# Attention and two feed-forward layers on one core: planes of probabilities in three buffers, casts and value products a step later

## What is computed

```python
scores = q @ k.T / sqrt(D) + bias(pos)     # per head
attn = exp(scores - max); attn = attn / (sum(attn) + 1e-9)
x = attn @ v                               # heads side by side: 2304 x 512
h = x @ w_in;  x = (s * relu(h)**2 + b) @ w_out
h = x @ w2_in; out = (h - tanh(h)) @ w2_out
```

## Time and profile before

| | us |
|---|---|
| median of 3 runs | 1117.99 |
| profiled execution | 1118.78 |
| its span | 1117.0 |
| TensorE matmul busy | 1055.4 (94%) |
| ScalarE busy | 728.8 (65%) |
| GpSimd (POOL) busy | 681.0 (61%) |
| VectorE busy | 622.2 (56%) |

### The profile page before, as it was taken

How to read it: one execution, slowest core, us unless ns; L and a number is a source line. 1 busy time by engine, 2 the same in 40 slices (tenths; PEclk the granted TensorE clock), 3 DMA queues, 4 the chain that set the end, 5 groups by cost and what they waited for, 6 DMA issues and landing times.

```text
span 1117.0 us, 16823 instructions
## 1 busy us (share of the span) xinstructions
PE 1055.4 (94%) x5668; PEld 912.4 (82%) x5668; DVE 622.2 (56%) x1120; ACT 728.8 (65%) x1477; POOL 681.0 (61%) x656
## 2 busy tenths in 40 slices
PE   4669999899999999999999999999999999999998
PEld 1158887778888888888888878888888888999998
DVE  6868876655775376458765754672361361450540
ACT  8968886666777587668776876784463463563552
POOL 1045674478678667767776778666455455555453
PEclk9989999999999999999999999999999999999999
DMA  4778875599779787988897899765333234333332
GB/s 164 248 237 254 282 212 143 146 223 252 207 189 263 220 202 198 260 201 208 225 247 187 208 229 236 209 159 142 115 97 114 94 114 131 112 113 113 95 122 81
DMA packets 185481, 202.49 MB, mean 181 GB/s; under 512 B 125954, under 2 KB 128692, under 8 KB 185396
## 3 DMA queue, kind: packets, MB, share of 16 engines
q1 hardware_dynamic: 185108, 201.35, 65.4%
q10 hardware_dynamic: 288, 0.07, 0.0%
HBM read 156.55 MB, written 15.64 MB: 154 GB/s over the span
## 4 chain that ended last, share of the span: by engine, by line
PE 58%; ACT 15%; issue 8%; DMA 8%; DVE 7%; SPq 2%; POOL 1%; ACTq 0%; DVEq 0%; POOLq 0%
PE ps_f L888 16%; PE ps_f L890 16%; PE ps_f L889 16%; DMA p_t<-planes 6%; ACT planes L608 3%; ACT x_raw L331 2%; DVE g_buf L948 2%; DVE g_buf L951 2%; ACT gh L901 1%; ACT ps_s L620 1%; PE ps_s L561 1%; ACT stage L348 1%; PE ps_o L520 1%; PE ps_o L535 1%; DVE planes L727 1%
## 5 line engine op out<-in xcount | busy, mean ns | idle before, releaser
L845 POOL TENSOR_TENSOR wl<-w_raw,wh 128x512 fp32r<-128x512 f32 x318 | 417.0, 1316 | 289.1 <-ACT wh L838 288.4
L888 PE MATMUL ps_f<-gh,wh 128*128 128x464 f32 (+1 forms) x640 | 243.1, 380 | 1.9 <-DVE g_buf L948 1.4
L888 PE MATMUL ps_f<-xh,wh 128*128 128x464 f32 (+1 forms) x640 | 241.0, 377 | 3.7 <-DVE g_buf L948 1.9
L890 PE MATMUL ps_f<-xh,wl 128*128 128x464 f32 (+1 forms) x640 | 237.7, 371 | 0.0
L889 PE MATMUL ps_f<-xl,wh 128*128 128x464 f32 (+1 forms) x640 | 237.5, 371 | 0.0
L889 PE MATMUL ps_f<-gl,wh 128*128 128x464 f32 (+1 forms) x640 | 237.3, 371 | 0.0
L890 PE MATMUL ps_f<-gh,wl 128*128 128x464 f32 (+1 forms) x640 | 237.1, 370 | 0.0
L838 ACT ACTIVATE wh<-w_raw 128x512 fp32r<-128x512 f32 x318 | 196.4, 623 | 45.7 <-PE ps_f L890 41.5
L888 PEld LDWEIGHTS ps_f<-xh,wh 128*128 128x128 f32 x640 | 120.7, 189 | 17.9 <-DVE g_buf L948 2.9
L888 PEld LDWEIGHTS ps_f<-gh,wh 128*128 128x128 f32 x640 | 120.9, 189 | 15.6 <-DVE g_buf L948 2.6
L890 PEld LDWEIGHTS ps_f<-xh,wl 128*128 128x128 f32 x640 | 120.4, 188 | 13.5
(11 more groups left out here) (107 smaller groups left out, 1695.5 us busy)
## 6 DMA issues: line engine op xcount, KB each, us to landing
w_raw<-in_w_out SPq DMA_DIRECT2D x80, 512.0 KB, 3.5
w_raw<-in_w_in SPq DMA_DIRECT2D x79, 512.0 KB, 3.5
bias_t<-bias_flat SPq DMA_DIRECT2D x128, 288.0 KB, 4.0
bias_flat<-stage SPq DMA_DIRECT2D x36, 295.5 KB, 2.2
k_raw<-in_kt SPq DMA_DIRECT2D x32, 288.0 KB, 3.9
q_raw<-in_qt SPq DMA_DIRECT2D x32, 288.0 KB, 3.5
v_raw<-in_vt SPq DMA_DIRECT2D x32, 288.0 KB, 3.3
bias_t<-bias_flat SPq DMA_DIRECT2D x32, 144.0 KB, 3.6
```

Source lines behind the costliest of these rows:

```text
L845: pool.tensor_tensor(wl[:, b % RING, :, :], raw_block(b), wh[:, b % RING, :, :].bitcast(F32), ALU.subtract).then_inc(w_lo_done, 1)
L888: pe.matmul(acc, hi, rhs_h[:, k0 + kk, 0:T], start=(first and kk == 0), stop=False)
L890: mm = pe.matmul(acc, lo, rhs_h[:, k0 + kk, 0:T], start=False, stop=(last and kk == 3))
```

## The change

- The scores of head 10 get SBUF homes, `p_even` and `p_odd`, in the space that the last rows of `gh` and `gl` take up later. Their planes are made in the step after, as for the other heads, and their scores wait for the row minimum alone.
- There are three plane buffers for the later heads: `planes` (two, over the dead `ptl`) and `plane_c` (over the dead `inv_b`). The low parts that head 9's tiles still need go to `ptl_late`, over `y`.
- `cast` and `valued` come a step later for tiles from 50 on, so there is one step more in all.
- SP sends the first plane of a head after all value products of head h - 2 but the last, and after the last cast of that head.
- RAW is 3: a third weight buffer. SP's loads run one pair further ahead, and a third pair is loaded at step (7, 2) of the part that runs alone.

```diff
RING = 4
-RAW = 2
+RAW = 3
 AHEAD = 3
...
     TILES = BH * NT
-    STEPS_AT = list(range(TILES + NT + 2))
+    STEPS_AT = list(range(TILES + NT + 3))
     FIRST = (H + 1) * NT + 1 + EXTRA
...
         p_lo_done = sem("p_lo_done")
-        plane_turned = [sem(f"plane_turned{i}") for i in range(2)]
+        plane_turned = [sem(f"plane_turned{i}") for i in range(3)]
         block_cast = sem("block_cast")
...
         pth = tile("pth", [P, 2, S], F32R)
-        ptl = tile("ptl", [P, 2, S], F32R)
+        with nc.sbuf_tensor("ptl", [P, 2, S], F32R) as ptl:
+            pass
+        planes = tile("planes", [P, 2, 2 * S], F16)
         o_tmp = tile("o_tmp", [D, 2, HALF])
...
         inv_row = tile("inv_row", [NT, P])
-        inv_b = tile("inv_b", [P, S])
+        with nc.sbuf_tensor("inv_b", [P, S], F32) as inv_b:
+            pass
+        plane_c = tile("plane_c", [P, 2 * S], F16)
         x_raw = tile("x_raw", [P, KD, RINGX])
...
             pass
+        with nc.sbuf_tensor("gh_head", [P, KF - 2, TMAX], F32), nc.sbuf_tensor("p_even", [P, S], F32) as p_even:
+            pass
         gh = tile("gh", [P, KF, TMAX], F32R)
+        with nc.sbuf_tensor("gl_head", [P, KF - 2, TMAX], F32), nc.sbuf_tensor("p_odd", [P, S], F32) as p_odd:
+            pass
         gl = tile("gl", [P, KF, TMAX], F32R)
+        with nc.sbuf_tensor("ptl_late", [P, 2, S], F32R) as ptl_late:
+            pass
         y = tile("y", [P, KD, TMAX])
...
-        planes = tile("planes", [P, 2, 2 * S], F16)
         def carve(home, parts):
...
-            if FIRST_PLANE <= g < FIRST_PLANE + NT:
-                return g
-            return g - 1 if FIRST_PLANE + NT < g <= TILES else None
+            return g - 1 if FIRST_PLANE < g <= TILES else None
+        def plane_home(f):
+            first = f - FIRST_PLANE
+            return first % 2 if first < 2 * NT else (first + 1) % 3
+        def plane_uses(home, f):
+            return len([e for e in range(FIRST_PLANE, f) if plane_home(e) == home])
...
-            return planes[:, f % 2, :]
+            home = plane_home(f)
+            return planes[:, home, :] if home < 2 else plane_c[:]
...
-            for par in range(2):
-                count = len([f for f in range(FIRST_PLANE, (n + 1) * NT) if f % 2 == par])
-                eng.wait_ge(plane_turned[par], count * DMA)
+            for home in range(3):
+                need(eng, plane_turned[home], plane_uses(home, (n + 1) * NT) * DMA)
...
             R = ROWS[i % NT]
-            return pth[P - R:P, slot(i), :] if R < P else ptl[:, slot(i), :]
+            return pth[P - R:P, slot(i), :] if R < P else low_parts(i)
+        def low_parts(i):
+            return (ptl if i < FIRST_PLANE - NT else ptl_late)[:, slot(i), :]
...
-            return g - NT - 1 if FIRST_PLANE <= g - NT - 1 < TILES else None
+            return g - NT - 2 if FIRST_PLANE <= g - NT - 2 < TILES else None
...
-            return g - NT - 2 if 0 <= g - NT - 2 < TILES else None
+            if g - NT - 2 < FIRST_PLANE:
+                return g - NT - 2 if g >= NT + 2 else None
+            return g - NT - 3 if FIRST_PLANE <= g - NT - 3 < TILES else None
...
                 if u < NT - 1:
-                    mm = pe.matmul(ps_o[:, half, 0:HALF], vhl[:, n % 2, u, :], ptl[:, slot(i), cols],
+                    mm = pe.matmul(ps_o[:, half, 0:HALF], vhl[:, n % 2, u, :], low_parts(i)[:, cols],
                                    start=False, stop=False)
...
                 pe.wait_ge(back_done, PACKS - 2 if t == 0 else PACKS)
-            elif n < TURNED or n == TURNED and t == 0:
+            elif n <= TURNED:
                 pe.wait_ge(min_done, n * NT + t)
-            elif n == TURNED:
-                pe.wait_ge(p_lo_done, t)
             else:
...
             need(pe, inv_row_done, v)
-            if v + 1 < TURNED:
-                pe.wait_ge(min_done, (v + 1) * NT + 3)
-            else:
-                pe.wait_ge(p_lo_done, 3)
+            pe.wait_ge(min_done, (v + 1) * NT + 3)
             pe.transpose(ps_s[0:NT, 0, HALF:HALF + P], inv[:], ident[:]).then_inc(inv_turned, 1)
...
-            return halves(p_t[:, n % 2, t, :]) if n < TURNED else score_bank(n, t)[:, :, 0:HALF]
+            if n < TURNED:
+                return halves(p_t[:, n % 2, t, :])
+            if n == TURNED:
+                return halves((p_odd if t % 2 else p_even)[:])
+            return score_bank(n, t)[:, :, 0:HALF]
...
             act.wait_ge(scale_done, f - FIRST_PLANE + 1)
-            need(act, plane_turned[f % 2], (f - FIRST_PLANE) // 2 * DMA)
+            need(act, plane_turned[plane_home(f)], plane_uses(plane_home(f), f) * DMA)
             act.activation(halves(plane(f)[:, 0:S]), score_home(n, t), ACT.Copy, scale=inv_n[:, t:t + 1])\
...
             f = planes_of(g)
-            if f is not None and f < g:
+            if f is not None:
                 act_plane(act, f)
...
                     .then_inc(sum_done, 1)
-                if f == g:
-                    act_plane(act, f)
             if t == 0 and turning(n):
...
             n, t = divmod(f, NT)
-            if f < FIRST_PLANE + 2:
-                dve.wait_ge(pv_done, FIRST_PLANE - NT - 1)
             dve.wait_ge(p_hi_done, f - FIRST_PLANE + 1)
...
             i, j, f = turned(g - alone), valued(g), planes_of(g)
-            if f is not None and f < g:
+            if f is not None:
                 dve_scale(dve, f)
...
                     .then_inc(min_done, 1)
-            if f == g:
-                dve_scale(dve, f)
             if f is not None:
...
                     else:
-                        sp.wait_ge(pv_done, (h - 1) * NT)
+                        sp.wait_ge(pv_done, (h - 1) * NT - 1)
+                        sp.wait_ge(block_cast, (h - 1) * NT - FIRST_PLANE)
                 R = ROWS[at]
                 sp.dma_start_transpose(turned_planes(h)[:, :, P * at:P * at + R], plane(f)[0:R, :])\
-                    .then_inc(plane_turned[f % 2], DMA)
+                    .then_inc(plane_turned[plane_home(f)], DMA)
             if t == 0 and turning(n - 1):
...
                 n, t = divmod(g, NT)
-                if t == 2 and n in (3, 5):
+                if t == 2 and n in (3, 5, 7):
                     sp_weights(sp, (n - 1) // 2)
```

## The result

The changed kernel takes 1100.09 us (median of 4 runs, 1098.85 to 1102.39), where the kernel before took 1117.94 beside it: a ratio of 0.9844, interval 0.9823 to 0.9865. That is 17.9 us less; 24 were forecast. The profiled execution took 1100.6 us, its span 1098.8.

A forecast was written before the change was run, and what follows sets the result against it. TensorE was taken to lose 34 us, in head 10's serial chain and in dense stretches waiting for landings and casts. Gains 9 + 16 less 0.5 (port) and 0.5 (SP) made 24: 1094 us, own range 1090 to 1099, wide range 1088 to 1107.

The forecast's parts named there:

- Head 10: Five row-minimum intervals of VectorE take 44.23 us where 33.4 would do; 9 of the 10.9 us gained, ends 6 and 10.9.
- The collision on VectorE: Head 10's second planes read two SBUF tiles, sharing ports with GpSimd: at most 3.9 us on VectorE, 0.5 charged.
- The dense stretches: Five stretches with attention steps between weight blocks: 16 of 20 us gained, bounds 6 and 20, limited by the DMA.
- The chain from ScalarE's wait at 338.06 to TensorE's at 346.04: ScalarE's 1.88 us landing wait makes wh, wl and POOL's cast late, so TensorE's value product waits 1.56 us.
- Three plane buffers: ScalarE overwrites a buffer after three steps, not two; its 35.3 us of landing waits, costing TensorE through others, should go.
- Casts a step later: First cast two steps after a head's last plane; POOL's 8.9 us of landing waits and TensorE's behind it go, cost nothing.
- The third weight buffer: Weight loads get two blocks (5 to 7 us) more slack; attention-only phase cost 0, bounds -0.5 to +2 us.
- SP's wait for the cast: SP's first plane of a head delayed 0.8 us per head; 0.5 us charged in all, bound 16 us.
- rival A: The DMA queue is the bound and buffers only move the wait; landings lengthen to 8 or 9 us: 1103, chance 0.15.

The follow-up runs named there:

- a1_head10: Changed kernel with everything but head 10's part taken back (two plane and two weight buffers, old cast and value steps, SP's old wait): 1109.8 us, ratio 0.9915.
- c1_before_light: Kernel before the change, loading only a quarter of each bias row from head 11 on (result not the reference's, for time alone): 1113.5 us, ratio 0.996.
- a4_cast_early: Changed kernel with casts and value products back in their old steps, three plane and three weight buffers kept: 1108.5 us, ratio 0.9911.
- b1_cast_first: Changed kernel with POOL's cast ahead of its split of k in the first step of a head: 1097.5 us, ratio 0.981.
- a2_two_planes: Changed kernel with two plane buffers in place of three: 1103.9 us, ratio 0.9866.
- b2_scale_late: Changed kernel with POOL's last scaling of two heads a step later, behind the first cast of head 10: 1099.2 us, ratio 0.9826.
- a3_raw2: Changed kernel with two weight buffers and the third early load left out: 1101.3 us, ratio 0.984.
- c2_after_light: Changed kernel, loading only a quarter of each bias row from head 11 on (for time alone): 1099.3 us, ratio 0.9827.

## Why the prediction was right, and where it was not

- **Head 10** was taken at 9 of 10.9 us; the book shows 10.7 gained with nothing kept back, and a1_head10 alone 11.1 in the book, 8.8 in time. Part of what was gained was the clock: before the change it stood at half for 3.4 us inside head 10, from 213.0 on. ScalarE and VectorE, forecast at a share of 0.80 and 0.78, are at 38.6 and 37.1 of 48.4 us, 0.80 and 0.77, in the first of the stretches shown. No score of head 10 waits. The collision on VectorE cost nothing on the path: the second planes of head 10 took 0.82, 0.82, 0.95, 0.82 and 1.18 us, 0.5 in all over the 0.82 of every other one, and the five intervals of the minimum are 33.7 us, 0.3 above 5 x 6.67. So the worst case that the prediction drew from the Trainium skill (page "SBUF — State Buffer", section "SBUF: two separate sides"), all five colliding for 3.4 us less gain, did not come about.
- **The dense stretches** were taken at 16 of 20 us and gave 6.8, near the low bound of 6. This is the term that was mis-sized. The prediction took "what is not due to planes or casts" as VectorE's 3.4 us only and called the other 20 landings. The runs split them otherwise: 5 us or more were landings (c1_before_light 5.0 at the least, a4_cast_early 6.1), 3.4 at block 53 and some 1.2 at block 22 POOL's order of its own work (b1_cast_first), 1.2 at block 19 POOL's scaling and split of q, and 3.5, at eight places, first value products behind VectorE's read of the output. The other 5 to 6 us are assigned to nothing. And the change itself added losses: 2.4 us at block 19 and, with twelve such first value products in place of eight, 1.9 there, so about 11 us went and 4.3 came (an estimate from the book's single blocks).
- **The chain from ScalarE's wait at 338.06 to TensorE's at 346.04** was read wrongly. The later cast and the wait of 1.5 us are there in the changed kernel without any wait of ScalarE for a landing. The rows had it: 3.35 us pass between the start of wl and the start of the cast, with wl itself 1.30. The two operations on k filled the rest (0.67 and 1.43 us), and that should have been asked.
- **Three plane buffers:** "the 35.3 us should go" was right, their price was not: 1.0 us in the book for 36.7 us of waits (a2_two_planes).
- **Casts a step later:** right, and the larger part, 6.1 us in the book and 7.5 to 8.4 in time. What the prediction left out is that this step moved the first cast of head 10 behind POOL's scaling, which made a loss of 3.6 us out of one of 1.2; 1.5 of the 3.6 is the clock (b2_scale_late, b1_cast_first).
- **The third weight buffer and SP's wait for the cast** were costed at nothing and at 0.5 us. a3_raw2 is 1.2 us above the changed kernel, 0.2 in the book. SP's wait was not undone by itself. It is longer than the 0.8 us per head at some heads, 7.9 us in 14 of 20, but with one wait for a transposed plane's landing in the whole run (1.3 us) nothing shows that it reached TensorE:

```profile
SPq L805 <- POOL pth L686: 7.9, 14, 2.8
```

- **The DMA as the next bound (rival A)** set the forecast at 16 in place of 20. The share did rise to 0.99 in two long stretches and 1.00 in a short one, as forecast (0.94 and 0.96 in the other two), but c2_after_light shows that it held nothing. Landings are a little longer, as A said (median 4.4 for 4.0 us), and late for one plane:

```profile
DMA to landing us min/median/max: 2.8/4.4/7.2
```

The forecast of 1094 was 6 us too low: 1 us outside its own range of 1090 to 1099 and inside the wide one, 1088 to 1107. Head 10 gave 1.7 us more than its term and the dense stretches 9.2 less. The mechanism held for head 10 and for the later casts; that the number was no further off owes something to luck, as the dense term was made smaller for a DMA bound that wasn't there. 1100 lies between the forecast and A's 1103, and came about by neither: what remained was POOL's order and VectorE's, not the queue.

## What to carry to other kernels

When a stretch is late against a count, put a cause on each late block before summing, and ask of a chain of waits what the engine did between the release and its late product; here 4.6 of the 8.8 us that stood under "waits for the cast" were still there when no landing was late, and all of it was other work queued ahead of the cast on the same engine. Where the profile names no engine ("issue"), take the waits in the code one by one and look which of them ended last. A wait of an engine that isn't the bound is worth what its consumer loses, not its length: 36.7 us of it cost 1.0. And after moving work by a step, look for what it now stands behind; POOL's order was worth nothing before the change and 2.6 us or somewhat more after it.

## What the runs showed of the hardware

- The DMA engines can be busy 0.94 to 1.00 of a stretch of 44 to 59 us without being its bound: with a quarter of the bias bytes from head 11 on, at a share of 0.85 to 0.91, each loss of the dense stretches but the clock's was the same to 0.1 us. A busy share alone doesn't tell that transfers are late.
- The granted clock fell to its lower level for 3.4 us behind 3.0 us in which TensorE was busy 1.25, in four of six kernels with the same stall. Where it fell, the loss was 3.6 us, where not, 2.0.
- VectorE's gl, with two inputs in SBUF, took 0.69 us at its shortest, 1.16 where its start fell 0.78 us into POOL's k2l (1.44 us), and 1.77 where it fell 0.15 us into it. A change of POOL's order moved TensorE's wait for g_buf from 0.67 to 1.33 us by it.
- The weight load of a head's first value product started 0.11 to 0.12 us after VectorE had read the bank, and the profile calls this wait "issue".
